# Attention with sums inverted after a transfer and spread by transfers, and a second chunk of keys weighted in fp16 halves made on VectorE

## Chip, cores and metric

The kernel runs on one core of one Trainium2 chip. The metric is the device time of one execution in microseconds (us); less is better.

## What is computed

Three stages follow one another; the output of each is the input of the next.

```python
def _attn_ref(q, k, v, g_q, g_k):           # q, k, v: (4, 12, 448, 64) fp32
    q_n, k_n = (rmsnorm(q, g_q), rmsnorm(k, g_k))
    scores = scale * np.matmul(q_n, k_n.transpose(0, 1, 3, 2))
    scores = scores - np.max(scores, axis=-1, keepdims=True)
    attn = np.exp(scores)
    attn = attn / (np.sum(attn, axis=-1, keepdims=True) + 1e-09)
    return np.matmul(attn, v)
def _moe_ref(x, w_gate, w_val, w_out):      # x: (1792, 768), d_ff 1536
    return 1.0 / (1.0 + np.exp(-(x @ w_gate))) * (x @ w_val) @ w_out
def _moe2_ref(x, w_gate, w_output_gate, w1, w2):   # 8 experts, F 1024, each token to its best one
    ...                                     # h = relu(x @ w1[e]); out = gate_w * eom * (h @ w2[e])
```

The change is in the first stage, the attention.

## The kernel before

The attention works on 24 pairs of heads (`PAIRS`), each with 448 queries and 448 keys (`S`), two heads of 64 dimensions (`D`) side by side in the 128 partitions. The keys of a pair are cut into an end of 64 keys, whose two heads lie together in one tile, and three chunks of 128 keys. Scores are turned: keys lie in the partitions, queries in the 448 columns, so the product with the values gives for each head 64 rows of output and, from columns of constants beside the values (`v_ones`), 64 equal rows that hold the sum of the exponentials.

Each engine has its own list of instructions, written out by hand in one loop over `STEPS`, and semaphores tie the lists together. In step n:

- TensorE forms the scores of pair n (`scores(n, 0)` for the end, then `scores(n, 1)` to `(n, 3)`; each is three fp16 products per head over 64 rows and one that adds the shift), the leading scores of pair n+1 for its row maxima (`leading(n+1, 0)` to `(n+1, 3)`), turns queries and keys of pair n+2 (`turn_qk`), turns the maxima of n+1 (`turn_max`), and weighs the values of pair n-1: `weigh_end(n-1)` for the end, in fp16 halves, and `weigh(n-1, h, ...)` for the three chunks, in fp32, one product per head and chunk. An fp32 product appears in the trace as two matmul records, so "x2" in a row is one product.
- ScalarE takes squares of pair n+4, exponentials (`exps(n, 0)` to `(n, 3)`), the high fp16 halves, and copies the outputs and sums out of PSUM (`take_out(n-2, 1)` at the step's start and `take_out(n-1, 0)` in its middle).
- VectorE makes the low fp16 halves (`v_low(n-1)`, line 954; `low_qk(n+2)`, lines 931 and 934), the reciprocal of the sums (`invert_sums(n-2)`, line 960, 128 x 448), four row maxima (`maxima`, line 940), the mean squares (`mean_squares(n+4)`, line 904) and the shift of the scores (`shift_rows(n+1)`, line 947).
- GpSimd finds the inverse root of the mean squares (`inverse_rms(n+3)`, lines 526 and 529, the latter a power) and applies it (`normalise(n+3)`, line 538), multiplies the output of pair n-2 by the inverted sums (`weigh_out`, line 545), makes the low half of the end's exponentials (`end_low(n)`, line 566) and the low half of the finished output (`x_low(n-2)`, line 549), which waits for ScalarE's `x_high(n-2)`, line 735; that follows `exps(n, 2)`.
- SyncE issues the loads of `qk` and `v`.

Waits that matter here: `scores(n+1, 0)` waits for `shift_rows(n+1)` and for `exps(n, 3)`; `leading(n+2, 0)` waits for both of `low_qk(n+2)`; `leading(n, 2)` and `(n, 3)` for the first and second maxima of n; `turn_max(n+1)` for the fourth; `weigh_end(n-1)` for `v_low(n-1)` and for the copies out of pair n-2. The lists are in strict order: an instruction that waits holds all behind it on its engine.

The first expert stage starts right behind: VectorE and SyncE wait there for all 24 pairs (`xt_ready`), while TensorE starts on the first batch; its third value group needs VectorE's first finished tile (`gated_ready`). Lines 1434, 1016, 1020, 1022 and 880 (`split_up`, of which a first call stands in VectorE's step 4) belong to this stage.

Of the kernel before, what the change touches and what calls it, by code (L numbers as in the profile page):

```python
# [6 lines left out]
F32 = mybir.dt.float32  # L7
# [49 lines left out]
def attention_moe_moe_kernel(nc, qk, v, v_last, g_qk, w_gate, w_val, w_out, w_out_t, router_w, out_gate_w,  # L57
# [19 lines left out]
    with ctx:  # L77
# [62 lines left out]
        x_raw = [at2.take(128, S, F32) for _ in range(2)]  # L140
        sums = [at2.take(128, S, F32) for _ in range(2)]
# [11 lines left out]
        tables = at2.take(PT, 2, F32)  # L153
        gains = at2.take(128, 2, F32)
# [87 lines left out]

        y_dram = nc.dram_tensor("y_parts", [N, 2 * DM], F16).ap()
# [34 lines left out]
        p_lo_ready = sem("p_lo_ready")  # L278
        v_hi_ready = sem("v_hi_ready")
# [5 lines left out]
        sums_inv_ready = sem("sums_inv_ready")  # L285
# [137 lines left out]
        STEPS = range(PAIRS + 2)  # L423
# [4 lines left out]
        def _(sp):  # L428
# [30 lines left out]
            for n in range(4, PAIRS + 5):  # L459
                if 3 <= n - 5:  # L460
                    load_v(n - 5)
                if has(n):
                    load_qk(n)
# [57 lines left out]
        def _(pool):  # L521
# [19 lines left out]
            def weigh_out(n):  # L541

                pool.wait_ge(sums_inv_ready, n + 1)
                pool.wait_ge(o_taken, 4 * n + 4)
                nc.gpsimd.tensor_tensor(x_out[n % 2], x_raw[n % 2], sums_inv[n % 2], ALU.mult).then_inc(x_ready, 1)
# [105 lines left out]
        def _(act):  # L651
# [54 lines left out]
            def exps(n, i):  # L706

                act.wait_ge(scores_ready, 4 * n + i + 1)
                if i == 0:
                    nc.scalar.activation(p_end[n % 2], ps[:, 2 * SCORE_SLOT, SQ], ACT.Exp, bias=lift[:, 0:1]).then_inc(probs_ready, 1)  # L710
                else:
                    nc.scalar.activation(probs[n % 2][:, :, i - 1], ps_pair(SCORE_SLOT, 128), ACT.Exp, bias=lift[:, 1:2])\  # L712
                        .then_inc(probs_ready, 1)
# [6 lines left out]
            def v_high(n):  # L720

                act.wait_ge(v_loaded[n % 3], 64 * (n // 3) + 64)
                nc.scalar.activation(v_parts[n % 2][:, 0], v_end[n % 3], ACT.Copy, scale=S_OP).then_inc(v_hi_ready, 1)

            def take_out(n, h):

                act.wait_ge(o_ready, 2 * n + h + 1)
                wait(act, x_ready, n - 1)
                o_rows, sum_rows = slice(h * D, (h + 1) * D), slice((1 - h) * D, (2 - h) * D)
                nc.scalar.activation(sums[n % 2][o_rows], ps[sum_rows, 6 + h, SQ], ACT.Copy, bias=1e-9 * S_OP).then_inc(o_taken, 1)  # L730
                nc.scalar.activation(x_raw[n % 2][o_rows], ps[o_rows, 6 + h, SQ], ACT.Copy).then_inc(o_taken, 1)
# [5 lines left out]
            act.wait_ge(lift_ready, 2)  # L737
            act.wait_ge(scratch_ready, 1)
# [12 lines left out]
            for n in STEPS:  # L751
                if n == 1:
                    load_up_weights()
                if n == 2:
                    load_router()
                if n == 4:
                    split_up(0, 0)
                if n == 6:
                    turned_high(0)
                if has(n - 2):  # L760
                    take_out(n - 2, 1)
                if has(n):
                    exps(n, 0)
                if has(n + 4):
                    take_squares(n + 4)
                if has(n):
                    end_high(n)
                    exps(n, 1)
                if has(n - 1):
                    take_out(n - 1, 0)  # L770
                if has(n):
                    exps(n, 2)
                if has(n - 2):
                    x_high(n - 2)
# [92 lines left out]
        def _(dve):  # L867
# [83 lines left out]
            def v_low(n):  # L951

                dve.wait_ge(v_hi_ready, n + 1)
# [30 lines left out]
            for n in STEPS:  # L984
# [8 lines left out]
                if has(n - 2):  # L993
# [285 lines left out]
        def _(pe):  # L1279
# [70 lines left out]

            def weigh(n, h, cs):

                if h == 0 and cs[0] == 0:
# [23 lines left out]
            for n in STEPS:  # L1377
# [4 lines left out]
                if has(n - 1):  # L1382
                    weigh_end(n - 1)
                    weigh(n - 1, 0, (0,))
# [11 lines left out]
                if has(n - 1):  # L1396
                    weigh(n - 1, 1, (0,))
# [201 lines left out]
```

## Time and profile before

| | |
|---|---|
| median of 3 runs | 1143.47 us (1142.17 to 1146.43) |
| the profiled execution | 1139.88 us, its span 1138.1 us |
| busy in the span | TensorE 97%, VectorE 52%, ScalarE 37%, GpSimd 23% |
| attention | from 0 to about 300 us |
| granted clock of TensorE, mean | 0.99 |

The profile is one execution of the kernel. Its page gives the busy share of each engine and the costliest groups; the trace behind it can be asked for the instructions of any stretch in order of time, for the chain of work that ended last, and for the transfers. All times in rows are microseconds from the start of the span. "L960" is line 960 of the kernel. PE is TensorE, DVE VectorE, ACT ScalarE, POOL GpSimd, SP SyncE. A row of consecutive equal instructions is merged, with their number behind an x.

### The profile page before, as it was taken

What the parts mean: (1) busy time and instruction counts of PE and PEld (TensorE: products, weight loads), DVE (VectorE), ACT (ScalarE), POOL (GpSimd) and SP (SyncE); (2) the same over time, 40 slices, a digit from 0 to 9 for tenths busy, and PEclk for the clock granted to TensorE, in tenths of its full rate; (3) what the DMA queues carried; (4) which work ended last, traced back from release to release, by engine and by line L of the source; (5) the groups of instructions that cost most, each with busy time, mean ns of one, the idle gap of its engine ahead of it and who ended that gap; (6) DMA issues with size and microseconds to landing.
All of it is one profiled execution on the core that took longest, in us unless ns stands there. A gap on an engine that the chain in (4) does not pass through costs nothing.

```text
span 1138.1 us, 17823 instructions
## 1 busy us (share of the span) xinstructions
PE 1100.3 (97%) x6617; PEld 573.3 (50%) x6618; DVE 594.7 (52%) x837; ACT 425.9 (37%) x631; POOL 256.5 (23%) x235
## 2 busy tenths in 40 slices
PE   7989999999999999999999999999898999999996
PEld 3434444444455555555555555556454555555554
DVE  7888888887433443333343300015656565556721
ACT  5768777777511111211111200001535253353510
POOL 4756767672200000000000000000211122112211
PEclk9999999999999999999999999999899999999999
DMA  5412222210121111111100501000848355366400
GB/s 144 122 49 62 61 65 58 66 25 17 60 67 56 56 55 55 55 55 55 55 28 1 195 28 41 28 32 23 296 163 319 118 211 206 108 217 225 142 20 18
DMA packets 71978, 104.11 MB, mean 91 GB/s; under 512 B 29310, under 2 KB 47870, under 8 KB 71920
## 3 DMA queue, kind: packets, MB, share of 16 engines
q1 hardware_dynamic: 63680, 89.84, 24.0%
q0 software_dynamic: 3120, 11.02, 2.7%
q10 hardware_dynamic: 5120, 2.48, 0.8%
q8 instruction: 36, 0.59, 0.2%
q14 instruction: 22, 0.18, 0.0%
HBM read 93.88 MB, written 13.76 MB: 95 GB/s over the span
## 4 chain that ended last, share of the span: by engine, by line
PE 87%; ACT 4%; DVE 4%; issue 2%; DMA 2%; ACTq 0%; POOL 0%; DVEq 0%; POOLq 0%; SPq 0%
PE ps L1434 29%; PE ps L1449 15%; PE ps L1528 12%; PE ps L1357 10%; PE ps L1506 7%; PE ps L1336 5%; PE ps L1316 2%; ACT arena L815 2%; DVE arena L1042 2%; PE ps L1348 2%; PE ps L1299 2%; PE ps L1338 1%; DMA arena<-in_moe_w 1%; PE ps L1515 1%; PE ps L1493 1%
## 5 line engine op out<-in xcount | busy, mean ns | idle before, releaser
L1434 PE MATMUL ps<-arena 128*128 128x448 f16 x1728 | 328.8, 352 | 0.0
L1434 PEld LDWEIGHTS ps<-arena 128*128 128x128 f16 x1728 | 168.1, 98 | 155.7
L1449 PE MATMUL ps<-arena 128*128 128x392 f16 (+1 forms) x1008 | 167.3, 329 | 2.4 <-DVE arena L1022 2.4
L1506 PE MATMUL ps<-arena 128*128 128x512 f16 x648 | 150.5, 388 | 5.6 <-DVE arena L1229 5.6
L1042 DVE SCALAR_TENSOR_TENSOR arena<-arena 128x768 f16<-128x768 f32 (+1 forms) x112 | 113.1, 1066 | 74.1 <-ACT arena L815 74.0
L1528 PE MATMUL ps<-arena 128*128 128x384 f16 x864 | 143.3, 326 | 4.0 <-DVE arena L1234 3.6
L1449 PEld LDWEIGHTS ps<-arena 128*128 (+1 forms) x1008 | 98.4, 98 | 70.4 <-DVE arena L1022 2.8
L1357 PE MATMUL ps<-arena 128*128 128x448 f32 x288 | 133.0, 573 | 0.0
L785 ACT ACTIVATE arena<-ps 128x448 f32<-128x448 f32 x48 | 26.1, 543 | 263.0 <-PE ps L1434 263.0
L1016 DVE SCALAR_TENSOR_TENSOR arena<-ps,arena 128x448 f32<-128x448 f32 x48 | 30.0, 624 | 176.0 <-PE ps L1434 96.1
L1528 PEld LDWEIGHTS ps<-arena 128*128 128x128 f16 x864 | 83.5, 98 | 58.6 <-issue 2.5
L940 DVE TENSOR_REDUCE arena<-ps 112x2 f16<-112x896 f32 x96 | 99.2, 1076 | 18.6 <-PE ps L1316 18.5
L815 ACT ACTIVATE arena<-arena 128x768 f16<-128x768 f32 (+1 forms) x112 | 97.5, 929 | 27.6 <-DMA arena<-in_moe_w 23.7
L1506 PEld LDWEIGHTS ps<-arena 128*128 128x128 f16 x648 | 63.7, 100 | 80.1 <-DVE arena L1229 6.4
L712 ACT ACTIVATE arena<-ps,arena 128x896 f32<-128x896 f32 x72 | 72.5, 1007 | 33.3 <-PE ps L1338 33.3
L960 DVE RECIPROCAL arena<-arena 128x448 f32<-128x448 f32 x24 | 70.8, 2951 | 10.3 <-ACT arena L730 10.3
L1336 PE MATMUL ps<-arena 64*128 64x448 f16 (+1 forms) x576 | 72.0, 356 | 3.0 <-ACT arena L712 1.7
L620 POOL MEMSET arena<- 128x1536 f16 x1 | 1.4, 1377 | 324.1 <-PE ps L1434 324.1
L835 ACT ACTIVATE arena<-ps,arena 128x384 f32<-128x384 f32 x36 | 18.9, 576 | 141.4 <-PE ps L1528 141.4
L1357 PEld LDWEIGHTS ps<-arena 128*128 128x128 f32 x288 | 47.6, 191 | 45.5 <-issue 45.5
L802 ACT ACTIVATE arena<-ps 128x768 f16<-128x768 f32 x14 | 11.3, 810 | 144.0 <-PE ps L1449 144.0
L1076 DVE TENSOR_SCALAR arena<-ps 128x16 f32 (+1 forms) x12 | 2.1, 171 | 119.9 <-ACT arena L802 119.9
(170 smaller groups left out, 1078.7 us busy)
## 6 DMA issues: line engine op xcount, KB each, us to landing
arena<-in_moe_w SPq DMA_DIRECT2D x48, 512.0 KB, 6.3
arena<-in_moe_w SPq DMA_DIRECT2D x64, 384.0 KB, 3.9
arena<-in_qk SPq DMA_DIRECT2D x23, 448.0 KB, 3.5
y_parts<-arena SPq DMA_DIRECT2D x16, 384.0 KB, 2.3
arena<-in_v SPq DMA_DIRECT2D x48, 96.0 KB, 2.6
arena<-in_moe_w_out SPq DMA_DIRECT2D x12, 384.0 KB, 5.5
arena<-in_w_out_t SPq DMA_DIRECT2D x11, 384.0 KB, 3.1
arena<-in_moe_w_gate SPq DMA_DIRECT2D x10, 384.0 KB, 4.2
```

What stands on the lines that cost most here:

```text
L712: nc.scalar.activation(probs[n % 2][:, :, i - 1], ps_pair(SCORE_SLOT, 128), ACT.Exp, bias=lift[:, 1:2])\
L815: nc.scalar.activation(hi, raw_rows(e, p), ACT.Copy, scale=S_OP).then_inc(w_hi_ready, 1)
L940: nc.vector.tensor_reduce(neg_max[n % 2][:, :, j], ps_pair(max_slot(n, j)), AX_X, ALU.max, negate=True)\
L960: nc.vector.reciprocal(sums_inv[n % 2], sums[n % 2]).then_inc(sums_inv_ready, 1)
L1016: nc.vector.scalar_tensor_tensor(gated[b % 2], ps[:, 2 * (b % 2) + 1, 0:S], 1.0 / S_OP, gate[b % 2], ALU.mult, ALU.mult).then_inc(gated_re ...
L1042: nc.vector.scalar_tensor_tensor(lo, raw_rows(e, p), S_OP, hi, ALU.mult, ALU.subtract).then_inc(w_lo_ready, 1)
L1336: nc.tensor.matmul(outs[h], qk_t[n % 3][rows, 1, kl, ks], qk_t[n % 3][rows, 0, ql], start=(kl + ql == 0), stop=False)
L1357: last = nc.tensor.matmul(ps[:, 6 + h, SQ], v_ones[n % 3][:, c, h * D:h * D + 2 * D], probs[n % 2][:, h, c], start=False, stop=(c == KCH - 1))
L1434: last = nc.tensor.matmul(ps[:, 2 * (b % 2) + g, 0:S], up_w[s][:, g, c, wl], xt[:, b * KC + c, xl], start=(c == 0 and wl + xl == 0), stop= ...
L1449: last = nc.tensor.matmul(ps[:, 4 + 2 * s + h, 0:cols], gt[:, f, gl, bass.ds(t * 128, 128)], wo[:, f, wl, h, 0:cols], start=(f == 0 and gl ...
L1506: last = nc.tensor.matmul(ps[:, b, :], x_t[:, xl, c], w1_s[s][:, c, wl, b * 512:(b + 1) * 512], start=(c == 0 and xl + wl == 0), stop=(c = ...
L1528: last = nc.tensor.matmul(ps[:, 4 + h, 0:HALF_DM], hid_t[:, b, hl, c], w2_s[s][:, k, wl, h * HALF_DM:(h + 1) * HALF_DM], start=(k == 0 and ...
```

## The change

For each pair, the sums are no longer inverted in all 64 equal rows of 448. One row per head is moved by a transfer into 64 rows of 7 (`move_sums`), VectorE inverts these 128 x 7 numbers, a transfer saves them to memory outside the core, and two transfers spread them over the 64 rows of each head again (`spread_inverse`). `weigh_out` and what follows it come one step later, and the buffers of `x_raw` and `sums` go from two to three.

The first of the three chunks of keys is weighed in fp16 halves as the end is: ScalarE makes the high half of its values (`v_high`), VectorE the low half (`v_low`, 128 x 192) and both halves of its exponentials (`first_split`, 128 x 896 each), and TensorE does three fp16 products in place of one fp32 one for each head (`weigh_first`). On VectorE `mean_squares` moves in front of the third and fourth maxima, and `invert_sums` and `first_split` stand behind them, in front of `shift_rows`. SyncE's loads of `qk` from pair 7 on and of `v` from pair 3 on go between the new transfers.

```diff
-        x_raw = [at2.take(128, S, F32) for _ in range(2)]
-        sums = [at2.take(128, S, F32) for _ in range(2)]
+        x_raw = [at2.take(128, S, F32) for _ in range(3)]
+        sums = [at2.take(128, S, F32) for _ in range(3)]
+        few_sums = [at2.take(128, S // D, F32) for _ in range(2)]
+        few_inv = [at2.take(128, S // D, F32) for _ in range(2)]
...
+        inv_dram = nc.dram_tensor("sums_inv", [2, 2, S], F32).ap()
...
-            for n in range(4, PAIRS + 5):
-                if 3 <= n - 5:
-                    load_v(n - 5)
-                if has(n):
-                    load_qk(n)
+            for n in range(4, 7):
+                load_qk(n)
+            def move_sums(n, h):
+                sp.wait_ge(o_taken, 4 * n + 2 * h + 1)
+                wait(sp, few_inv_ready, n - 1)
+                sp.dma_start(few_sums[n % 2][h * D:(h + 1) * D],
+                             sums[n % 3][h * D:h * D + 1].rearrange("o (p c) -> o p c", c=S // D)).then_inc(sums_moved, 16)
+            def spread_inverse(n):
+                sp.wait_ge(few_inv_ready, n + 1)
+                sp.dma_start(inv_dram[n % 2].rearrange("h (p c) -> (h p) c", c=S // D), few_inv[n % 2]).then_inc(inv_saved, 16)
+                wait(sp, x_ready, n - 1)
+                sp.wait_ge(inv_saved, 16 * n + 16)
+                for h in range(2):
+                    sp.dma_start(sums_inv[n % 2][h * D:(h + 1) * D], inv_dram[n % 2, h].unsqueeze(0).to_broadcast([D, S]))\
+                        .then_inc(inv_spread, 16)
+            for n in range(PAIRS):
+                move_sums(n, 0)
+                move_sums(n, 1)
+                if has(n + 7):
+                    load_qk(n + 7)
+                if has(n + 3):
+                    load_v(n + 3)
+                spread_inverse(n)
...
-                pool.wait_ge(sums_inv_ready, n + 1)
+                pool.wait_ge(inv_spread, 32 * n + 32)
...
-                if has(n - 2):
-                    weigh_out(n - 2)
+                if has(n - 3):
+                    weigh_out(n - 3)
                 if has(n):
                     end_low(n)
-                if has(n - 2):
-                    x_low(n - 2)
+                if has(n - 3):
+                    x_low(n - 3)
...
+                nc.scalar.activation(v_first[n % 2][:, 0], v_ones[n % 3][:, 0], ACT.Copy, scale=S_OP).then_inc(v1_hi_ready, 1)
...
+            def first_split(n):
+                dve.wait_ge(probs_ready, 4 * n + 2)
+                wait(dve, o_ready, 2 * (n - 1))
+                nc.vector.tensor_copy(p_first[n % 2][:, 0], probs[n % 2][:, :, 0]).then_inc(p1_hi_ready, 1)
+                dve.wait_ge(p1_hi_ready, n + 1)
+                nc.vector.tensor_tensor(p_first[n % 2][:, 1], probs[n % 2][:, :, 0], p_first[n % 2][:, 0], ALU.subtract)\
+                    .then_inc(p1_lo_ready, 1)
             def invert_sums(n):
-                dve.wait_ge(o_taken, 4 * n + 3)
-                wait(dve, x_ready, n - 1)
-                nc.vector.reciprocal(sums_inv[n % 2], sums[n % 2]).then_inc(sums_inv_ready, 1)
+                dve.wait_ge(sums_moved, 32 * n + 32)
+                wait(dve, inv_saved, 16 * (n - 1))
+                nc.vector.reciprocal(few_inv[n % 2], few_sums[n % 2]).then_inc(few_inv_ready, 1)
...
                     v_low(n - 1)
-                if has(n - 2):
-                    invert_sums(n - 2)
                 if has(n + 1):
                     maxima(n + 1, 0)
                     maxima(n + 1, 1)
+                if has(n + 4):
+                    mean_squares(n + 4)
                 if has(n + 1):
                     maxima(n + 1, 2)
                     maxima(n + 1, 3)
-                if has(n + 4):
-                    mean_squares(n + 4)
+                if has(n - 2):
+                    invert_sums(n - 2)
+                if has(n):
+                    first_split(n)
...
+            def weigh_first(n, h):
+                pe.wait_ge(v1_lo_ready, n + 1)
+                pe.wait_ge(p1_lo_ready, n + 1)
+                for pl, vl in PASSES:
+                    nc.tensor.matmul(ps[:, 6 + h, SQ], v_first[n % 2][:, vl, h * D:h * D + 2 * D], p_first[n % 2][:, pl, h],
+                                     start=False, stop=False)
...
-                    weigh(n - 1, 0, (0,))
+                    weigh_first(n - 1, 0)
...
-                    weigh(n - 1, 1, (0,))
+                    weigh_first(n - 1, 1)
```

## Rows read from the trace of the kernel before

**Rows 1.** Stretch of 40 us: busy of each engine, clock, DMA share, GB/s.

```profile
200.00:240.00 40.00, 39.69 (x240) 17.43 (x238) 35.52 (x38) 31.62 (x52) 28.45 (x21) 1.00 0.19 53
```

**Rows 2.** Chain that ended last, one step and more: start, length, what.

```profile
193.25 0.69 PE ps L1336 x6
...
194.12 0.33 PE ps L1316 x2
...
196.55 0.57 PE ps L1336 x6
...
199.00 0.52 PE ps L1316 x4
...
200.28 0.95 PE ps L1357 x2
...
203.01 1.57 PE ps L1357 x4
204.58 0.69 PE ps L1336 x6
```

**Rows 3.** VectorE in order of time, same step: start, length.

```profile
193.39 0.28 DVE L954 SCALAR_TENSOR_TENSOR arena<-arena 128x128 f16<-128x128 f32 x1
193.85 2.95 DVE L960 RECIPROCAL arena<-arena 128x448 f32<-128x448 f32 x1 [0.19 <-ACT arena L730]
...
199.38 2.09 DVE L940 TENSOR_REDUCE arena<-ps 112x2 f16<-112x896 f32 x2 [0.63 <-PE ps L1316]
201.38 1.21 DVE L904 TENSOR_REDUCE arena<-arena 112x16 f32<-112x1024 f32 x1
203.05 0.62 DVE L947 TENSOR_TENSOR arena<-ps,arena 128x448 f16<-128x448 f32 x1 [0.46 <-PE ps L1323]
...
204.19 0.61 DVE L934 TENSOR_TENSOR arena<-ps,arena 128x448 f16<-128x448 f32 x1
```

**Rows 4.** GpSimd in order of time, same step.

```profile
191.94 2.90 POOL L529 TENSOR_TENSOR arena<-arena 112x16 f32<-112x16 f32 x1
194.92 1.90 POOL L538 TENSOR_TENSOR arena<-arena 112x1024 f32<-112x1024 f32 x1
...
201.87 1.03 POOL L549 TENSOR_TENSOR arena<-arena 128x448 f16<-128x448 f32 x1 [2.86 <-ACT arena L735]
```

**Rows 5.** ScalarE in order of time, same step.

```profile
200.32 1.01 ACT L712 ACTIVATE arena<-ps,arena 128x896 f32<-128x896 f32 x1 [0.18 <-PE ps L1338]
...
202.99 0.31 ACT L723 ACTIVATE arena<-arena 128x128 f16<-128x128 f32 x1
203.19 1.01 ACT L712 ACTIVATE arena<-ps,arena 128x896 f32<-128x896 f32 x1
```

**Rows 6.** VectorE in order of time, step 4, last steps, next stage.

```profile
63.98 3.53 DVE L880 SCALAR_TENSOR_TENSOR arena<-arena 128x768 f16<-128x768 f32 x2 [0.80 <-ACT arena L656]
...
291.62 1.03 DVE L954 SCALAR_TENSOR_TENSOR arena<-arena 128x128 f16<-128x128 f32 x1 [4.71 <-ACT arena L723]
...
306.86 0.19 DVE L892 TENSOR_SCALAR arena<-ps 128x32 f32<-128x32 f32 x1 [2.97 <-POOL arena L549]
...
308.26 0.40 DVE L1020 CAST arena<-arena 128x448 f16<-128x448 f32 x1
308.69 0.62 DVE L1022 TENSOR_TENSOR arena<-arena 128x448 f16<-128x448 f32 x1
```

**Rows 7.** GpSimd in order of time, beside two rows of the last group.

```profile
64.64 2.06 POOL L538 TENSOR_TENSOR arena<-arena 112x1024 f32<-112x1024 f32 x1
...
291.46 1.03 POOL L549 TENSOR_TENSOR arena<-arena 128x448 f16<-128x448 f32 x1 [2.35 <-ACT arena L735]
```

**Rows 8.** TensorE in order of time, start of the first expert stage.

```profile
300.47 24.00 PE L1434 MATMUL ps<-arena 128*128 128x448 f16 x126
```

**Rows 9.** Line 450, loads of 64 rows of 256 bytes: issue, landing.

```profile
L450 SPq DMA_DIRECT2D arena<-in_v_last x48: 500/603/856, 4.5 to 274.5; - x48
...
DMA to landing us min/median/max: 2.0/2.4/6.8
```

More of the change, by code:

```diff
@@ L153, in attention_moe_moe_kernel @@
         tables = at2.take(PT, 2, F32)
+        p_first = [at2.take(128, 2 * 2 * S, F16).rearrange("p (l h s) -> p l h s", l=2, h=2) for _ in range(2)]
+        v_first = [at2.take(128, 2 * 3 * D, F16).rearrange("p (l c) -> p l c", l=2) for _ in range(2)]
         gains = at2.take(128, 2, F32)
@@ L278, in attention_moe_moe_kernel @@
         p_lo_ready = sem("p_lo_ready")
+        p1_hi_ready = sem("p1_hi_ready")
+        p1_lo_ready = sem("p1_lo_ready")
+        v1_hi_ready = sem("v1_hi_ready")
+        v1_lo_ready = sem("v1_lo_ready")
         v_hi_ready = sem("v_hi_ready")
@@ L284, in attention_moe_moe_kernel @@
         o_taken = sem("o_taken")
-        sums_inv_ready = sem("sums_inv_ready")
+        sums_moved = sem("sums_moved")
+        few_inv_ready = sem("few_inv_ready")
+        inv_saved = sem("inv_saved")
+        inv_spread = sem("inv_spread")
         x_ready = sem("x_ready")
@@ L421, in has @@
             return 0 <= n < PAIRS
-        STEPS = range(PAIRS + 2)
+        STEPS = range(PAIRS + 3)
         block = ctx.enter_context(nc.Block())
@@ L541, in weigh_out @@
             def weigh_out(n):
-                pool.wait_ge(sums_inv_ready, n + 1)
+                pool.wait_ge(inv_spread, 32 * n + 32)
                 pool.wait_ge(o_taken, 4 * n + 4)
-                nc.gpsimd.tensor_tensor(x_out[n % 2], x_raw[n % 2], sums_inv[n % 2], ALU.mult).then_inc(x_ready, 1)
+                nc.gpsimd.tensor_tensor(x_out[n % 2], x_raw[n % 3], sums_inv[n % 2], ALU.mult).then_inc(x_ready, 1)
             def x_low(n):
@@ L711, in exps @@
                 else:
-                    nc.scalar.activation(probs[n % 2][:, :, i - 1], ps_pair(SCORE_SLOT, 128), ACT.Exp, bias=lift[:, 1:2])\
+                    nc.scalar.activation(probs[n % 2][:, :, i - 1], ps_pair(SCORE_SLOT, 128), ACT.Exp,
+                                         bias=lift[:, 0:1] if i == 1 else lift[:, 1:2])\
                         .then_inc(probs_ready, 1)
@@ L727, in take_out @@
                 act.wait_ge(o_ready, 2 * n + h + 1)
-                wait(act, x_ready, n - 1)
+                wait(act, x_ready, n - 2)
                 o_rows, sum_rows = slice(h * D, (h + 1) * D), slice((1 - h) * D, (2 - h) * D)
-                nc.scalar.activation(sums[n % 2][o_rows], ps[sum_rows, 6 + h, SQ], ACT.Copy, bias=1e-9 * S_OP).then_inc(o_taken, 1)
-                nc.scalar.activation(x_raw[n % 2][o_rows], ps[o_rows, 6 + h, SQ], ACT.Copy).then_inc(o_taken, 1)
+                nc.scalar.activation(sums[n % 3][o_rows], ps[sum_rows, 6 + h, SQ], ACT.Copy, bias=1e-9 * S_OP).then_inc(o_taken, 1)
+                nc.scalar.activation(x_raw[n % 3][o_rows], ps[o_rows, 6 + h, SQ], ACT.Copy).then_inc(o_taken, 1)
             def x_high(n):
@@ L737, in _ @@
             act.wait_ge(lift_ready, 2)
+            act.wait_ge(ones_ready, 3)
             act.wait_ge(scratch_ready, 1)
@@ L772, in _ @@
                     exps(n, 2)
-                if has(n - 2):
-                    x_high(n - 2)
+                if has(n - 3):
+                    x_high(n - 3)
                 if has(n + 2):
@@ L951, in v_low @@
             def v_low(n):
+                dve.wait_ge(v1_hi_ready, n + 1)
+                nc.vector.scalar_tensor_tensor(v_first[n % 2][:, 1], v_ones[n % 3][:, 0], S_OP, v_first[n % 2][:, 0], ALU.mult, ALU.subtract)\
+                    .then_inc(v1_lo_ready, 1)
                 dve.wait_ge(v_hi_ready, n + 1)
@@ L992, in _ @@
                     v_low(n - 1)
-                if has(n - 2):
-                    invert_sums(n - 2)
                 if has(n + 1):
@@ L1349, in weigh_end @@
                                          start=(pl + vl == 0), stop=False)
+            def weigh_first(n, h):
[4 more added lines that the diff above has]
+                                     start=False, stop=False)
             def weigh(n, h, cs):
-                if h == 0 and cs[0] == 0:
+                if h == 0:
                     pe.wait_ge(v_loaded[n % 3], 64 * (n // 3) + 64)
```

## Prediction, made before the changed kernel was run

> **What bounds the kernel now.** I read the page first (the table above): TensorE is busy for 97% of the span, but that is a mean over four stages, and the change touches the attention stage only, the first 300 us. The table by stretches [rows 1] shows TensorE busy 39.69 of 40 us there at the full granted clock (1.00, the 2.4 GHz level), VectorE 35.52 (89%), ScalarE 31.62, GpSimd 28.45. The chain of waits [rows 2] shows what a step costs: from one `scores(n, 0)` at 193.25 to the next at 204.58 is 11.33 us, and every piece of the chain is TensorE. So a step is as long as TensorE's own list, and the question is whether that stays so when the list gets shorter.
>
> I measure the step from two marks. "L" is the start of `leading(n+1, 2)`, 199.00. "Lead" is the start of `leading(n+1, 0)`, 194.12. From Lead to L TensorE needs 4.88 us, from L to the next Lead (194.12 + 11.33 = 205.45) 6.45 us.
>
> VectorE's list [rows 3] runs beside it: the second pair of maxima starts at 199.38 (L + 0.38) and is over when line 904 starts (L + 2.38); `shift_rows` starts at L + 4.05, the two of `low_qk` follow, and the last of them ends at 204.19 + 0.61 = L + 5.80. Lead waits for it and comes at L + 6.45, so 0.65 us are to spare [rows 2, 3]. This loop (L, maxima, shift, low, Lead) is the second bound, and the change puts work right into it.
>
> **The change, part by part.**
>
> *TensorE.* Two fp32 products a step (each shown as x2, 0.95 us [rows 2], the one in the row and its twin for the other head) become three fp16 ones each over all 128 rows. Back to back such a product takes 24.00 / 126 = 0.19 us [rows 8], three 0.57. The 0.95 has 0.16 in it for the switch from products over 64 rows, since two in a row behind products of full height (203.01) take 1.57. For fp16 I take 0.10, near the 0.12 by which line 1336's six products last longer behind the fp32 ones (193.25, 0.69) than behind their own kind (196.55, 0.57). That is 0.67 a head, 0.28 saved, 0.56 a step; bounds 0.28 and 0.38 a head. If nothing else changed: 10.77 us a step.
>
> *VectorE, taken away.* The reciprocal over 448 columns, 2.95 us [rows 3], in 24 steps. It stands in front of the first maxima, not between L and Lead, so its 2.95 us were filled time and never in the second loop. It gives that loop nothing. `mean_squares` (1.21) also moves out from between the maxima and the shift; it was followed by an idle 0.46 us, and the time from the maxima to the shift (1.67) comes free.
>
> *VectorE, added.* A reciprocal over 7 columns: no such row; the nearest, 32 columns, took 0.19 [rows 6], bound above 0.28 (line 954, 128 columns). I take 0.20. The cast of 896 columns: 448 took 0.40 [rows 6], which is a fixed 0.16 and two columns a cycle, so 0.62; bound above 1.09 at one a cycle. The subtraction of 896 columns: 448 took 0.62 at one column a cycle (0.47 and 0.15), so 1.09. These three stand between the last maxima and the shift: cast from L + 2.58 to 3.20, subtraction from 3.24 to 4.33. Then shift (0.54 to the next start), low (0.60), low (0.61 to its end): 6.00; with 0.11, an allowance, until TensorE runs, Lead at L + 6.11. TensorE's own list would bring it at 6.45 - 0.28 = 6.17. Undisturbed, the second loop just fits: 0.06 us to spare. The extra `v_low` over 192 columns (0.35, next start after 0.27) falls behind Lead, in front of `weigh_end`, and takes the place of a 0.08 us wait there.
>
> *What disturbs it.* GpSimd's `x_low` starts at 201.87 = L + 2.87 [rows 4], because it follows ScalarE's `exps(n, 2)`, which starts 1.55 us earlier at the end of `scores(n, 2)` [rows 5]. All of this hangs on the same place in TensorE's list, so in the changed kernel too it starts at L + 2.87, in the middle of the cast. Two places of this trace show what then happens. At 63.98 two `split_up` subtractions (each 768 columns and 0.15 by the arithmetic above, 0.95) took 3.53 us together [rows 6]: GpSimd's multiplication began at 64.64, 0.29 us before the first was over, and ran 2.06 instead of 1.90 [rows 4] to 66.70 [rows 7]; the second subtraction ended at 67.51, that is 0.80 us (768 columns) and 0.01 behind it. At 291.62 a `v_low` that takes 0.28 took 1.03: `x_low` ran from 291.46 to 292.49 and it ended 0.16 later. So a VectorE instruction that reads two tensors of the arena waits until GpSimd's is over, and GpSimd, when it queued first, goes in between two of VectorE's. Here: `x_low` ends at 2.87 + 1.03 + 0.20 = L + 4.10; the subtraction ends 0.93 + 0.03 later, at 5.06, instead of 4.33; shift, low, low: 6.73; Lead at L + 6.84. From Lead to L: 4.88 - 0.28 - 0.08 = 4.52. Step: 11.36 us, against 11.33. What TensorE's list gives, the collision takes.
>
> The Trainium skill says the same in its page "SBUF — State Buffer", section "Who interferes with whom": an instruction of VectorE with two SBUF inputs and one of GpSimd that reads SBUF exclude each other for their whole length, and the one that issues first goes. For `x_low` the rows agree (0.28 became 1.03). For GpSimd's power (line 529) they don't: it runs 2.90 us from 191.94, `v_low` at 193.39 lies inside it and took 0.28 [rows 3, 4]. By the page alone the two `v_low` would wait for the power too, some 0.3 us more a step, 6 us in all; the measurement decides, and I leave it out of the sum.
>
> *ScalarE.* `v_high` has one more copy, 192 columns beside the 128 that took 0.31 [rows 5]: 0.27 us more before `exps(n, 3)`. That ended at 204.20 and the next `scores` starts at 204.58, so 0.38 covers it, with 0.11 left. Without that cover it would cost 0.27 a step.
>
> *GpSimd.* The same instructions, the last two for a pair one step older. From `x_low`'s end at L + 4.10: line 526 (0.3 with its gaps), power 2.90, normalise 1.90 and their gaps: `weigh_out` can start at about L + 9.4.
>
> *SyncE and the transfers.* Five issues more in a step. Per pair: `few_inv` at L + 2.8, saved after one transfer, spread by two after another. No row has such a transfer; the nearest, 64 rows of 256 bytes, lands 2.4 us after its issue and takes 0.6 to issue [rows 9] (from 2.0 to 6.8 over its 48). So 2.8 + 2.4 + 0.6 + 2.4 = L + 8.2, 1.2 us before `weigh_out` wants it. Queued behind the waiting save are the next moves of sums; these land near L - 1.6 of the next step and are wanted at L + 2.4. Loads of `qk` and `v` in the same queue wait for things that are past by then, and are used a step later. All hidden.
>
> *Start and end.* The sums over the 24 pairs: some 19 steps at + 0.03: + 0.6. Four steps in which no `x_low` or no maxima stand in the way gain the 0.56: - 2.2. Step 0, where TensorE waits for VectorE anyhow, gets 1.7 us of split, of which I count 1.3 (bounds 0 and 1.7). Steps 4 to 6, where VectorE also splits the first weights, have the longer `v_low` on the path: + 1.0. In the tail, the last pair's reciprocal (2.95) gives way to three transfers and a short one, some 5.5 us more; VectorE's next stage began at 306.86 [rows 6] and gave its first tile 1.4 us later, while TensorE had work from 300.47 that waits for this tile only after five groups of 18 products, 17.1 us, at 317.6 [rows 8]. With the delay the tile comes at about 313.7, and 3.9 us of cover are left. Nothing is paid. Sum: + 0.7 us on the profiled 1139.88 us (span 1138.1). The median of the runs shown is 1143.47, 3.6 above it; on the median: **1144 us**.
>
> **The rivals.**
>
> *No collision that counts* (VectorE's subtraction follows its cast at once, and GpSimd waits). Then the step is TensorE's list, 10.77. For it: the two are only 0.04 us apart. Against it: at 64.64 GpSimd came in between two that were closer. 22 steps at - 0.56 and the 2.3 of start: - 10, 1133 us.
>
> *The transfers come late* (slower). If the spread lands later than L + 9.4, `weigh_out` and `end_low` slip; later than about L + 11.9, that is if each of the two legs takes 4.3 us and not 2.4, `end_low` lies on the cast as well. Then cast and subtraction each wait for one of GpSimd's, about 1 us more a step: + 20, 1164 us. For it: the longest landing of that row was 6.8. Against it: 1.8 us of slack a leg, and the transfer engines are 19% busy there [rows 1].
>
> *The lock of the skill's page also for the power*: + 6, 1150 us; against it stands the row named above.
>
> **How the numbers follow.** The collision at about my price 0.5, no collision 0.28, late transfers 0.13, the power too 0.09. The first has its own range of 1137 to 1151: 0.1 us a head less on TensorE is - 4, the subtraction 0.2 to 0.3 longer held is + 4 to + 6. A measurement of this kernel tells about 0.5% (5.7 us) from no change. Faster than 1137.8: the second case, and some 0.08 of the first, 0.35. Slower than 1149.2: late transfers, half of the power's, and 0.06 of the first, 0.24. The same: 0.41. The range, 1131 to 1159, leaves out some of the late transfers and the far end of the gain.
>
> **What would show it.** Right: in a step near 200 us, TensorE with two idle places of together 0.5 to 0.6 us, before `scores(n+1, 0)` released by the shift and before `leading(n+2, 0)` released by `low_qk`; the 896-column subtraction near 1.8 us in place of 1.09, ending right behind GpSimd's `x_low` plus its own columns; step length 11.3 to 11.4. Wrong in the second way: subtraction 1.09, `x_low` near 2 us, step 10.8. Wrong in the third: GpSimd idle before `weigh_out`, released by a transfer. What would fell the whole: a cast at one column a cycle, or three fp16 products that take 0.95.

## Result and the profile after

The changed kernel takes 1147.48 us (median of 20 runs, 1144.19 to 1149.61), the kernel before 1143.72 us in the same comparison (20 runs, 1139.7 to 1146.6). The ratio is 1.0032, 95% interval 1.0023 to 1.0042: slower by 0.3%, 2.6 to 4.8 us, which is less than the 0.5% taken as the bound of "the same". The profiled execution took 1147.05 us, its span is 1145.3 us.

The same stretch of 40 us as in [rows 1], of the kernel after; the columns are those of that group:

```profile
200.00:240.00 40.00, 38.50 (x245) 16.75 (x244) 35.36 (x47) 32.27 (x56) 30.57 (x23) 1.00 0.28 74
```

TensorE was busy 39.69 us of 40 there and is now busy 38.50. The stretch holds a little more work than before all the same, because a step got shorter by 0.05 us: `scores(n, 0)` now starts every 11.28 us. The rows of TensorE in order of time show the step and its two waits; the first and third row are the starts of two neighbouring steps, the second is L (200.68), the last is Lead:

```profile
194.95 0.76 PE L1388 MATMUL ps<-arena 64*64 64x448 f16 x6 [0.19 <-DVE arena L985]
...
200.68 0.59 PE L1368 MATMUL ps<-arena 64*112 64x448 f16 x4
...
206.23 0.76 PE L1388 MATMUL ps<-arena 64*64 64x448 f16 x6 [0.19 <-DVE arena L985]
...
207.44 0.40 PE L1368 MATMUL ps<-arena 64*112 64x448 f16 x2 [0.27 <-DVE arena L972]
```

The 0.19 us is the wait for `shift_rows` (line 985 now), the 0.27 the wait for `low_qk` (line 972). Before, both places had none. VectorE in order of time, beside [rows 3]:

```profile
201.11 2.09 DVE L978 TENSOR_REDUCE arena<-ps 112x2 f16<-112x896 f32 x2 [0.57 <-PE ps L1368]
203.12 0.19 DVE L1010 RECIPROCAL arena<-arena 128x7 f32<-128x7 f32 x1
203.23 0.57 DVE L1002 CAST arena<-arena 128x896 f16<-128x896 f32 x1
203.84 1.81 DVE L1004 TENSOR_TENSOR arena<-arena 128x896 f16<-128x896 f32 x1
205.56 0.61 DVE L985 TENSOR_TENSOR arena<-ps,arena 128x448 f16<-128x448 f32 x1
...
206.69 0.61 DVE L972 TENSOR_TENSOR arena<-ps,arena 128x448 f16<-128x448 f32 x1
```

GpSimd in order of time, beside [rows 4]; line 584 is `x_low`, 561 the first instruction of `inverse_rms`, 564 the power, 580 `weigh_out`:

```profile
203.61 1.08 POOL L584 TENSOR_TENSOR arena<-arena 128x448 f16<-128x448 f32 x1 [2.13 <-ACT arena L772]
204.78 0.93 POOL L561 TENSOR_SCALAR arena<-arena 112x16 f32<-112x16 f32 x1
205.79 2.90 POOL L564 TENSOR_TENSOR arena<-arena 112x16 f32<-112x16 f32 x1
...
210.62 1.14 POOL L580 TENSOR_TENSOR arena<-arena 128x448 f32<-128x448 f32 x1
```

`x_low` starts at 203.61, in the middle of the cast (203.23 to 203.80), and ends at 204.69. The subtraction of 896 columns starts at 203.84 and ends at 205.65, that is 0.96 us behind `x_low`. Its own length is 1.09 (shown below). In these rows line 978 is the maxima, 1010 the short reciprocal, 1002 the cast, 1004 the subtraction, 985 `shift_rows`, 969 and 972 `low_qk`. The chain of waits says the same; between two pieces of TensorE it now runs through VectorE's maxima, cast, subtraction, shift and low halves, where [rows 2] has TensorE alone:

```profile
200.75 0.34 PE ps L1368 x2
...
205.56 0.61 DVE arena L985
206.18 0.59 DVE arena L969
206.77 0.54 DVE arena L972
...
207.44 0.40 PE ps L1368 x2
...
208.56 0.67 PE ps L1408 x3
```

The transfers, from the table of issues (number, size of each, median time from issue to landing):

```profile
arena<-sums_inv SPq DMA_DIRECT2D x48, 112.0 KB, 2.7
...
arena<-arena SPq DMA_DIRECT2D x48, 1.8 KB, 2.2
...
sums_inv<-arena SPq DMA_DIRECT2D x24, 3.5 KB, 1.5
```

### The profile page after: what moved, and what is told of

Read it like the earlier page. It is cut to its first block, busy times and chain, and to the rows that moved or that the text cites. A ratio compares the mean times of both kernels' runs of the same rounds, so it can differ in the third digit from the quotient of the medians.

```text
span 1145.3 us, 18269 instructions
## 1 busy us (share of the span) xinstructions
PE 1088.4 (95%) x6665; PEld 568.5 (50%) x6666; DVE 592.5 (52%) x909; ACT 431.2 (38%) x655; POOL 272.2 (24%) x235
## 4 chain that ended last, share of the span: by engine, by line
PE 76%; DVE 11%; issue 6%; DMA 3%; ACT 3%; POOL 0%; DVEq 0%; ACTq 0%; POOLq 0%; SPq 0%
PE ps L1494 29%; PE ps L1509 15%; PE ps L1588 12%; PE ps L1566 7%; PE ps L1417 4%; DVE arena L978 3%; PE ps L1368 2%; ACT arena L853 2%; DVE arena L1094 2%; PE ps L1388 2%; PE ps L1408 2%; DMA arena<-in_moe_w 2%; PE ps L1400 2%; DVE arena L969 1%; DVE arena L985 1%
## 5 line engine op out<-in xcount | busy, mean ns | idle before, releaser
L1588 PE MATMUL ps<-arena 128*128 128x384 f16 x864 | 146.1, 330 | 8.1 <-DVE arena L1286 7.7
L978 DVE TENSOR_REDUCE arena<-ps 112x2 f16<-112x896 f32 x96 | 102.8, 1094 | 36.0 <-PE ps L1368 34.1
L1417 PE MATMUL ps<-arena 128*128 128x448 f32 x192 | 83.9, 559 | 0.0
L564 POOL TENSOR_TENSOR arena<-arena 112x16 f32<-112x16 f32 x21 | 61.0, 2903 | 1.8
L650 POOL DMA_INDIRECT out<-arena x18 | 23.1, 1282 | 149.5 <-ACT arena L873 149.5
```

What stands on the lines that cost most here:

```text
L564: nc.gpsimd.tensor_tensor(rms_inv, rms_sq, minus_half, ALU.pow).then_inc(rms_inv_ready, 1)
L978: nc.vector.tensor_reduce(neg_max[n % 2][:, :, j], ps_pair(max_slot(n, j)), AX_X, ALU.max, negate=True)\
L1417: last = nc.tensor.matmul(ps[:, 6 + h, SQ], v_ones[n % 3][:, c, h * D:h * D + 2 * D], probs[n % 2][:, h, c], start=False, stop=(c == KCH - 1))
L1588: last = nc.tensor.matmul(ps[:, 4 + h, 0:HALF_DM], hid_t[:, b, hl, c], w2_s[s][:, k, wl, h * HALF_DM:(h + 1) * HALF_DM], start=(k == 0 and ...
```

## The experiments

Each is an edit of the changed kernel, or of none. Beside each median stands that of the kernel before on the same chip and the ratio of the two.

**The order on the shared ports, by one wait.** `x_low_waits`:

```diff
             def x_low(n):
+                pool.wait_ge(p1_lo_ready, min(n + 4, PAIRS))
                 pool.wait_ge(x_hi_ready, n + 1)
```

> The changed kernel with one wait more: GpSimd's x_low also waits for the subtraction of first_split of the same step. Theory (the two exclude each other and x_low goes first): the 896-column subtraction takes 1.09 us instead of 1.80, x_low starts behind it, TensorE no longer waits for the shift and at most 0.1 us for low_qk, a step is 10.8 us instead of 11.28; over some 19 steps 9 us less than the changed kernel, about 1138. Rival (the subtraction is slow by itself, or VectorE's list between maxima and shift is simply too long): subtraction stays at 1.8 us, a step stays at 11.28 or gets longer by GpSimd's delay, 1147 to 1150.

Measured 1137.25 us against 1143.79, ratio 0.9937 (0.9918 to 0.9956). VectorE, then GpSimd, then TensorE of this kernel in order of time (line 1003 is the cast, 1005 the subtraction, 585 `x_low`, 1389 `scores`):

```profile
195.09 0.58 DVE L1003 CAST arena<-arena 128x896 f16<-128x896 f32 x1
195.71 1.09 DVE L1005 TENSOR_TENSOR arena<-arena 128x896 f16<-128x896 f32 x1
196.71 0.61 DVE L986 TENSOR_TENSOR arena<-ps,arena 128x448 f16<-128x448 f32 x1
```

```profile
196.87 1.04 POOL L585 TENSOR_TENSOR arena<-arena 128x448 f16<-128x448 f32 x1 [2.41 <-DVE arena L1005]
198.00 0.20 POOL L561 TENSOR_SCALAR arena<-arena 112x16 f32<-112x16 f32 x1
```

```profile
187.14 0.76 PE L1389 MATMUL ps<-arena 64*64 64x448 f16 x6
...
197.92 0.76 PE L1389 MATMUL ps<-arena 64*64 64x448 f16 x6
...
198.79 0.40 PE L1369 MATMUL ps<-arena 64*112 64x448 f16 x2
```

With a wait added, and no work taken away, the subtraction takes 1.09 us instead of 1.80, the two waits of TensorE are gone and a step is 197.92 - 187.14 = 10.78 us. That is TensorE's list: 0.55 us under the 11.33 of before, where the prediction had 0.56. So the subtraction isn't slow by itself, and VectorE's list isn't too long: what lengthens the step is the 0.71 us in which the subtraction is held behind `x_low`. The wait moves GpSimd's later work too, and in step 4 that is worth more than in a quiet step (shown further down). Line 561 shows the other side: 0.20 us here, 0.93 in the changed kernel, where it started at 204.78 while the subtraction ran to 205.65.

**The subtraction where GpSimd is at its power.** `subtraction_last`:

```diff
-                if has(n - 1):
-                    v_low(n - 1)
...
                 nc.vector.tensor_copy(p_first[n % 2][:, 0], ...).then_inc(p1_hi_ready, 1)
+            def first_rest(n):
                 dve.wait_ge(p1_hi_ready, n + 1)
...
                 if has(n + 2):
                     low_qk(n + 2)
+                if has(n):
+                    v_low(n)
+                    first_rest(n)
```

`v_low` moves from the start of a step to the end of the step before, and the subtraction behind it.

> The changed kernel with another order on VectorE: the cast stays behind the maxima, then shift_rows, low_qk, v_low of the same pair (moved ahead from the next step), and the 896-column subtraction last, when GpSimd is at its power. Theory: a two-input instruction inside the power isn't held, so the subtraction takes 1.09 us there, nothing on the path to the next leading scores is held, and a step is TensorE's list, 10.7 to 10.8 us: 9 to 11 us less than the changed kernel, 1137. If GpSimd's power held it too (as a whole-length lock would have it), the subtraction takes 1.5 us or more, weigh_first waits for it and a step is 11.0 to 11.3.

Measured 1136.37 us against 1143.79, ratio 0.9928 (0.9907 to 0.9949); steps of 10.78 us. VectorE (line 1007 is the subtraction) and GpSimd's power in order of time:

```profile
197.44 0.62 DVE L985 TENSOR_TENSOR arena<-ps,arena 128x448 f16<-128x448 f32 x1 [0.71 <-PE ps L1379]
...
199.57 1.08 DVE L1007 TENSOR_TENSOR arena<-arena 128x896 f16<-128x896 f32 x1
```

```profile
197.99 2.90 POOL L564 TENSOR_TENSOR arena<-arena 112x16 f32<-112x16 f32 x1
```

The subtraction lies from 199.57 to 200.65, wholly inside the power (197.99 to 200.89), reads two tensors of the arena and takes 1.08 us. So the power, unlike `x_low`, doesn't hold this instruction. By the rule of the Trainium skill that the prediction quotes (page "SBUF — State Buffer", section "Who interferes with whom") it would have; the subtraction now says what `v_low` said in [rows 3, 4], and the measurement decides.

**Each half alone.** `transfers_only` leaves the first chunk in fp32 and keeps the transfers, the later `weigh_out` and VectorE's order; `halves_only` keeps the fp16 halves and has the reciprocal over 448 columns in its old place.

```diff
-                if has(n):
-                    first_split(n)
...
-                    weigh_first(n - 1, 0)
+                    weigh(n - 1, 0, (0,))
```

> Only the first half of the change: sums folded, inverted and spread by transfers, everything one step later, VectorE's order as in the changed kernel, but the first chunk of keys in fp32 as before. Theory: the 2.95 us reciprocal was filled time beside a full TensorE, so a step stays at 11.33 us and the attention ends where it ended (300.2 us, within 0.5). If the transfers or the added tensor in memory are what makes the expert stages of the changed kernel some 3 us longer, the total is 1146 to 1147; if they are innocent, 1143 to 1144.

Measured 1145.22 us against 1143.79, ratio 1.0013 (0.9999 to 1.0026): no measurable difference. A step is 11.33 us, as before: taking 2.9 us a step away from an engine that stood beside a full TensorE gave nothing. Two things came out otherwise than expected: the attention ended at 302.5 us, not at 300.2 within 0.5 (step 4 took 17.68 us, and one unchanged profile of before has 17.61 there), and the total lies between the two ranges that I had set, so this run doesn't tell whether the transfers lengthen the later stages.

```diff
-                dve.wait_ge(sums_moved, 32 * n + 32)
-                wait(dve, inv_saved, 16 * (n - 1))
-                nc.vector.reciprocal(few_inv[n % 2], few_sums[n % 2]).then_inc(few_inv_ready, 1)
+                dve.wait_ge(o_taken, 4 * n + 3)
+                wait(dve, x_ready, n - 1)
+                nc.vector.reciprocal(sums_inv[n % 2], sums[n % 2]).then_inc(few_inv_ready, 1)
```

> Only the second half of the change: the first chunk in fp16 halves, the reciprocal over 448 columns back in its old place, no transfers. Theory: VectorE's list from one leading scores to the next is then v_low 0.5, reciprocal 2.9, four maxima 4.0, mean squares 1.1, cast 0.6, subtraction 1.0, shift 0.5, low 1.2 and 0.1 to restart, with no x_low in the way: 11.8 to 12 us a step, VectorE the bound, total 1152 to 1158. Rival (TensorE's shorter list decides): 10.8 us a step, 1135.

Measured 1163.88 us against 1143.79, ratio 1.0182 (1.0157 to 1.0208); a step is 12.42 us. I expected 11.8 to 12.0 with no `x_low` in the way, and a total of 1152 to 1158: both missed. VectorE, then GpSimd (line 976 cast, 978 subtraction, 984 reciprocal, 558 `x_low`):

```profile
192.88 0.61 DVE L976 CAST arena<-arena 128x896 f16<-128x896 f32 x1
193.52 1.81 DVE L978 TENSOR_TENSOR arena<-arena 128x896 f16<-128x896 f32 x1
...
197.37 2.94 DVE L984 RECIPROCAL arena<-arena 128x448 f32<-128x448 f32 x1
```

```profile
192.64 1.74 POOL L558 TENSOR_TENSOR arena<-arena 128x448 f16<-128x448 f32 x1 [2.55 <-ACT arena L746]
```

`x_low` is in the way here too: the subtraction takes 1.81, 0.7 us more than alone. VectorE has no idle place in this step, so the hold adds its full length: without it the step would be about 11.7 (an estimate, 12.42 - 0.72). So the halves alone make VectorE the bound, the transfers alone give nothing, and only together they could shorten the step. The gain of the pair is 1163.88 - 1147.48 = 16.4 us for the transfers, given the halves.

**How late may the transfers come.** `late_spread`:

```diff
-                sp.dma_start(inv_dram[n % 2]...., few_inv[n % 2]).then_inc(inv_saved, 16)
+                for k in range(3):
+                    sp.dma_start(inv_dram[n % 2]...., few_inv[n % 2]).then_inc(inv_saved, 16)
+                    sp.wait_ge(inv_saved, 48 * n + 16 * k + 16)
...
```

> The changed kernel with the save of the inverted sums made three times over, one after the other, so that the spread starts two round trips (2.27 us each in the changed kernel's trace) later and lands about 4.5 us later, at 12.7 us behind leading(n+1, 2) instead of 8.2; GpSimd is ready for weigh_out at 9.9. Theory of the slack: the first 1.7 us cost nothing, the other 2.8 push weigh_out and end_low, and end_low then lies on the cast of first_split as x_low lies on the subtraction: about 1 us more a step, 12.2 to 12.4 instead of 11.28, total 1165 to 1172. Rival (transfers have room to spare in every direction): no change, 1147 to 1149.

Measured 1164.39 us against 1143.64, ratio 1.0185 (1.0162 to 1.0209). VectorE, GpSimd and TensorE (line 1003 cast, 1005 subtraction, 581 `weigh_out`, 602 `end_low`, 585 `x_low`, 1389 `scores(n, 0)`):

```profile
200.25 1.14 DVE L1003 CAST arena<-arena 128x896 f16<-128x896 f32 x1
201.43 1.80 DVE L1005 TENSOR_TENSOR arena<-arena 128x896 f16<-128x896 f32 x1
```

```profile
199.78 1.13 POOL L581 TENSOR_TENSOR arena<-arena 128x448 f32<-128x448 f32 x1 [2.65 <-DMA arena<-sums_inv]
200.87 1.42 POOL L602 TENSOR_TENSOR arena<-arena 128x448 f16<-128x448 f32 x1
202.25 1.88 POOL L585 TENSOR_TENSOR arena<-arena 128x448 f16<-128x448 f32 x1
```

```profile
203.97 0.75 PE L1389 MATMUL ps<-arena 64*64 64x448 f16 x6 [1.30 <-ACT arena L748]
```

`weigh_out` waits 2.65 us for the spread and lies on the cast, which takes 1.14 instead of 0.58 and ends at 201.39, 0.48 behind it. `end_low` lies on the subtraction, which takes 1.80 and ends at 203.23, 0.94 behind it. `x_low` comes after both and is itself held by the subtraction (1.88 instead of 1.03). So it is GpSimd's instruction before the expected one that each of VectorE's two waits for. The step that ends at 203.97 is 12.25 us long.

The total, 1164.39, is the price of the second rival, 1164, but it lies just under the 1165 to 1172 expected for this run, and not every step pays. Steps 7 to 22 last between 11.18 and 13.12 us, and the last six of them 11.18 to 11.32. There too the spread is late, for instance:

```profile
234.85 1.14 POOL L581 TENSOR_TENSOR arena<-arena 128x448 f32<-128x448 f32 x1 [1.58 <-DMA arena<-sums_inv]
```

`weigh_out` is over at 235.99, when the cast starts; this step ends at 239.04 and lasts 11.18 us. So 1.58 us of lateness cost nothing and 2.65 us cost 1 us. The lateness itself isn't the constant 4.5 us that I had set: near 200 us the spread lands about 14.9 us behind L (184.89 to 199.78), not 12.7, because SyncE works off its own list in order and the repeated saves held up all behind them: this pair's save began at 189.87, 5.0 behind L, not 2.8.

One thing I had not seen: TensorE's wait of 1.30 is released by ScalarE, whose `x_high` waits for `weigh_out` with `exps(n, 3)` queued behind it.

**Where the rest of the difference is.** The attention of the first two profiles differs by 0.7 us (first product of the next stage at 300.5 and 301.2), the medians by 3.8. Five runs bear on that: each kernel unchanged for two further profiles, and `dram_behind`, with the two tensors in memory declared in the other order.

```diff
-        inv_dram = nc.dram_tensor("sums_inv", [2, 2, S], F32).ap()
         y_dram = nc.dram_tensor("y_parts", [N, 2 * DM], F16).ap()
+        inv_dram = nc.dram_tensor("sums_inv", [2, 2, S], F32).ap()
```

> The changed kernel with its small tensor in memory declared behind y_parts, the tensor that the expert stage gathers rows from, and not ahead of it. The attention of the changed kernel ends only 0.7 us later than before, yet its median is 3.8 us above. If the shifted address of y_parts is what slows the gathers and loads of the last stage, the total falls by some 3 us, to 1144 to 1145; if it is the spread of the last stage from run to run or something that the order doesn't touch, it stays at 1147 to 1148. Attention as in the changed kernel: 11.28 us a step.

> The kernel before, unchanged, for a second profile. The attention should end at 300.5 us within 0.5 again; the last stage, from its first product to the end, took 324.3 us in the first profile and should differ by several us, since the profiled run was 3.6 us under the median.

> The changed kernel, unchanged, for a second profile. Steps of 11.28 us again; the attention ends at 301.2 us within 0.5; the last stage took 331.1 us in the first profile: if 3 us of the difference to before are the run's chance, it is anywhere from 326 to 333 here.

> The kernel before, a third profile, to tell the last stage's spread (324.3 and 330.4 us so far, from its first product to its last) from a difference between the kernels. Attention ends at 300.5 us.

> The changed kernel, a third profile, for the same reason (331.1 and 331.7 us so far). If the last stage is longer by 3 us in the changed kernel itself it is 330 to 333 again and the kernel before's is 326 to 329; if it is chance, the two overlap. Attention ends between 301 and 303.5 us.

`dram_behind` measured 1148.92 us against 1144.27, ratio 1.0048 (1.0032 to 1.0063): the order isn't it. The profiles, in us:

| | attention ends | last stage | total of that run |
|---|---|---|---|
| before | 300.5, 300.4, 302.0 | 324.3, 330.4, 328.2 | 1139.88, 1147.59, 1145.32 |
| after | 301.2, 303.2, 302.8 | 331.1, 331.7, 331.0 | 1147.05, 1149.67, 1148.68 |
| after, tensors in the other order | 302.2 | 328.7 | 1145.71 |

The last stage (from its first to its last product) has the same instructions in both kernels. TensorE in order of time, `before_third` and then `after_third`:

```profile
818.25 1.46 PE L1493 MATMUL ps<-arena 128*128 128x128 f16 x12 [3.92 <-DMA arena<-y_parts,arena]
...
873.22 9.35 PE L1528 MATMUL ps<-arena 128*128 128x384 f16 x48 [3.82 <-DVE arena L1234]
```

```profile
819.91 0.84 PE L1553 MATMUL ps<-arena 128*128 128x128 f16 x12 [3.02 <-DMA arena<-y_parts,arena]
...
874.45 10.73 PE L1588 MATMUL ps<-arena 128*128 128x384 f16 x48 [4.17 <-DVE arena L1286]
```

It waits for gathered rows and, indirectly, for weights from memory, and by other amounts in each run. The attention's mean rose by 1.4 us (301.0 to 302.4), the last stage's by 3.6 (327.6 to 331.3) where the single runs spread over 6 us in the kernel before (324.3 to 330.4). So a part of the 3.8 us is the attention's, and the larger part lies in a stage that the change doesn't touch. By the bounds set for the third profiles (330 to 333 against 326 to 329 would speak for the kernel) 331.0 and 328.2 point to the changed kernel, but the 330.4 of `before_again` doesn't fit, and the other profiles of this case, all of edits of the changed kernel, have 327.7 to 332.0. Whether that part is a property of the changed kernel or of which runs were profiled, these profiles don't settle; the cause stays open.

A piece of the attention's rise can be named. The order in step 1 is the same in all three profiles of the changed kernel, and TensorE waits 1.97, 1.97 and 1.83 us for the shift at its start. In the first one the granted clock stayed at 1.00 behind the wait; in the two others it was 0.50, the 1.2 GHz level, from 32 to 33 us, and the same products took longer. `after`, then `after_again`:

```profile
31.36 0.74 PE L1400 MATMUL ps<-arena 64*128 64x448 f16 x6
```

```profile
31.78 1.35 PE L1400 MATMUL ps<-arena 64*128 64x448 f16 x6
```

Step 1 lasted 11.10 us in the first, 12.28 and 12.15 in the others.

**A version that beats both.** `weights_spread` is `subtraction_last`, with the split of the first expert weights no longer done at once in step 4:

```diff
-                if n == 4:
-                    split_up(0, 0)
+                if n in (5, 6):
+                    dve.wait_ge((up_half_ready, up_hi_ready)[n - 5], 1)
+                    half = nc.vector.scalar_tensor_tensor(up_w[0][:, n - 5, :, 1], up_raw[0][:, n - 5], S_OP,
+                                                          up_w[0][:, n - 5, :, 0], ALU.mult, ALU.subtract)
```

> The version with the subtraction last, and the first gate and value weights split one half per step in steps 4 to 6 (ScalarE behind end_high, VectorE at the step's start) instead of both at once in step 4, router and turned weights two steps later. Steps 4 to 7, which took 12.95, 13.72 and 11.37 us there against 10.78 in a quiet step, should come to 10.8 to 11.3 each: 4 to 5 us less, 1131 to 1133. If the halves at the step's start are held by GpSimd or hold up the maxima, the gain is under 2 us.

Measured 1132.86 us (11 runs, 1127.87 to 1144.03) against 1144.27, ratio 0.9919 (0.9894 to 0.9943). The edit also moves ScalarE's halves of that split, and the router's and turned weights two steps later. Its profile has steps 4 to 7 at 10.79, 10.78, 10.78 and 10.78 us, and the attention ends at 283.1 us, 17.4 before that of the first profile of before and 7.5 before that of `subtraction_last` (290.6). The total fell by less, 11.4 us, and varies more from run to run. Its ratio overlaps that of `subtraction_last` (0.9907 to 0.9949), so the totals don't show the 7.5 us: both beat the kernel before, and which of the two is better stays open. In its profile the last stage takes 330.9 us, 3.3 above the mean of the three profiles of before.

## Why the prediction held, point by point

The forecast was 1144 us and no measurable change, with the reason that a collision takes what TensorE's list gives. Measured: 1147.48, within the range of the likeliest case. The mechanism of the step is shown; the size of the total is in part luck, as the last points say.

- *TensorE, 0.56 us a step.* 0.55 (`x_low_waits`). Right.
- *The reciprocal was filled time.* Right (`transfers_only`, 11.33).
- *The list from L to Lead.* Forecast and measured, from L: cast 2.58 and 2.55 (203.23 - 200.68), its length 0.62 and 0.57, end of the subtraction 5.06 and 4.97, end of `low_qk` 6.73 and 6.62, Lead 6.84 and 6.76. Step 11.36 and 11.28. The 0.1 us comes from `x_low`: I let it lose 0.20 us to the cast, it lost 0.05 (1.08 instead of 1.03).
- *`x_low` goes in between.* Right, and shown by one wait.
- *The power holds nobody.* Right for the two instructions that lay inside it, `v_low` and the subtraction (`subtraction_last`).
- *Transfers hidden.* Forecast landing L + 8.2; measured 205.61 + 0.55 + 2.7 = L + 8.2, the second spread's issue and landing. `weigh_out` starts at L + 9.9 behind GpSimd's own work.
- *The start.* Step 0 lasts 10.31 us instead of 8.89: 1.4, forecast 1.3. Steps 1 to 3 last 11.10, 10.78 and 10.96 us instead of 11.74, 11.53 and 11.33: 1.8 us gained, where the prediction had 2.2 for four steps, one of them at the end. That gain is the first profiles' alone: over three profiles each, steps 1 to 3 take 34.2 us before and 33.6 after, a gain of 0.7. The lower clock in step 1, told above, is the larger part of what is missing; the sum had no term for it. The fourth of these steps is the end: from `scores(23, 0)` to the next stage the attention takes 16.0 us instead of 17.2 (first profiles), but step 22 takes 11.28 instead of 10.78, together 0.7 us.
- *Steps 4 to 6: the term that was mis-sized.* Forecast + 1.0 us, measured + 2.5 (18.16, 11.82, 12.14 against 16.45, 11.33, 11.86). VectorE, GpSimd and TensorE in step 4 of the kernel after (lines 992 and 995 are `v_low`):

```profile
65.43 3.14 DVE L992 SCALAR_TENSOR_TENSOR arena<-arena 128x192 f16<-128x192 f32 x1
68.50 1.11 DVE L995 SCALAR_TENSOR_TENSOR arena<-arena 128x128 f16<-128x128 f32 x1
```

```profile
65.14 2.13 POOL L573 TENSOR_TENSOR arena<-arena 112x1024 f32<-112x1024 f32 x1
67.24 1.12 POOL L580 TENSOR_TENSOR arena<-arena 128x448 f32<-128x448 f32 x1
68.32 1.14 POOL L601 TENSOR_TENSOR arena<-arena 128x448 f16<-128x448 f32 x1
```

```profile
69.67 1.30 PE L1400 MATMUL ps<-arena 64*128 64x448 f16 x6 [5.45 <-DVE arena L995]
```

The extra `v_low` of 0.35 us took 3.14: normalise held it first, and `weigh_out`, queued behind, went next. It ended at 68.57, 0.21 us after `weigh_out`. Then `end_low` held the second one. I had costed the new instruction at its length, in the one step where it lies on GpSimd's two-tensor work; it was held twice, and its neighbour once more. Over steps 4 to 6 the kernels with that split at once take, above three steps of their own plain length: 42.12 - 3 x 11.28 = 8.3 us in the changed kernel (8.8 and 8.4 in its other profiles); 39.64 - 3 x 11.33 = 5.7 before (5.5 and 6.8 in the others); and 37.42 - 3 x 10.78 = 5.1 in `x_low_waits`. That last run has `v_low` at the same place as the changed kernel, so it isn't the place that costs: there `x_low` waits, all of GpSimd's list comes later, and `v_low` is through before normalise starts:

```profile
66.48 0.35 DVE L993 SCALAR_TENSOR_TENSOR arena<-arena 128x192 f16<-128x192 f32 x1
```

```profile
66.82 1.98 POOL L573 TENSOR_TENSOR arena<-arena 112x1024 f32<-112x1024 f32 x1
```

So the one added wait frees two collisions, the subtraction's in every step and `v_low`'s in step 4. `subtraction_last` also has 38.04 - 3 x 10.78 = 5.7, but from another place: in its step 5 an instruction of the router (line 912, 128 x 96, 0.26 us in the changed kernel) took 3.92 us across three of GpSimd's. In `weights_spread` these steps are 10.79, 10.78 and 10.78. A part of the prices before and after is TensorE's clock: behind its wait in step 4 (3.61 and 5.45 us) the granted clock was 0.50 from 70 to 71 us in both, and 1.00 in `subtraction_last`, where it waited 1.22 us.

- *The tail.* VectorE entered the next stage at 311.26 instead of 306.86, 4.4 us later where 5.5 was forecast, and TensorE ran its first 126 products in 24.00 us without a gap, as in [rows 8]. Hidden, as said.
- *What the sum had no term for.* The last stage. The sum for the attention was + 0.7 us, and the first profile after shows + 0.7. That agreement is luck: the errors of its parts nearly cancel (1.5 too little in steps 4 to 6, 0.08 too much in each of some 15 steps), and the mean of three profiles each is + 1.4. The remaining 2.4 us of the 3.8 are outside it, and why the last stage was longer stays open.

## What to carry to other kernels

When an engine's work is moved off a full engine onto another, draw up the loop that the receiving engine closes (here: maxima, shift, low halves, next scores) and put beside it, at the same marks, what GpSimd does at that moment; in these rows a two-tensor instruction of VectorE costs its length plus the rest of GpSimd's where that is `x_low`, `end_low`, `weigh_out` or normalise, and its length alone beside the power. Where two such lists collide, try the order before the work: one added wait took 10 us off. And a half of a change that gives nothing alone (the transfers) can be what makes the other half affordable.

## What the runs showed of the hardware that was not expected

- A short instruction can lose several times in a row: 0.35 us became 3.14 behind two of GpSimd, and 0.26 us became 3.92 behind three (`subtraction_last`, 78.70), each of which was queued there and went next.
- The cast, which reads one tensor, is held too: 1.14 us instead of 0.58 behind `weigh_out` (`late_spread`).
- A wait of one length doesn't give one clock: behind the same 1.97 us of idle TensorE the granted clock was 1.00 in one profile of a kernel and 0.50 in the next.
- The hold works on small ones too: a 112 x 16 instruction of GpSimd took 0.93 us instead of 0.20 behind VectorE's subtraction.
- The recorded start of a GpSimd instruction needn't be the moment from which it holds the other. In `halves_only` `x_low` starts at 192.64, the cast starts 0.24 us later and still takes 0.61, near its plain 0.58, and it is `x_low` that stretches to 1.74.
- A transfer of one row of 1792 bytes into 64 rows of 28 lands after 2.2 us, one of 128 rows of 28 bytes to memory after 1.5, and one that spreads a row over 64 rows after 2.7.
